# A fused attention and expert kernel: attention steps ordered one deeper, GpSimd's value loads ahead of its stores, squares in pairs, key copies on ScalarE

## What is computed

```python
def _attn_ref(q, k, v):                      # (4, 8, 576, 64) each
    B, H, S, D = q.shape
    window, dilation, scale = 32, 4, 1.0 / np.sqrt(D)
    scores = scale * np.matmul(q, k.transpose(0, 1, 3, 2))
    pos = np.arange(S)
    rel = pos[:, None] - pos[None, :]
    mask_plain = (rel >= 0) & (rel < window)
    mask_dil = (rel >= 0) & (rel < window * dilation) & (rel % dilation == 0)
    masks = np.stack([mask_plain if h < H // 2 else mask_dil for h in range(H)], axis=0)
    scores = np.where(masks[None, :, :, :], scores, -1000000000.0)
    attn = np.exp(scores - np.max(scores, axis=-1, keepdims=True))
    attn = attn / (np.sum(attn, axis=-1, keepdims=True) + 1e-09)
    return np.matmul(attn, v)

x = attention, as rows (2304, 512)
x = moe(x)      # xn = x / norm of the row; expert = argmax(xn @ en.T / tau);
                # gate * relu(x @ w1[e]) @ w2[e]
out = (h * cos(h)) @ w_out, with h = x @ w_in
```

## Time and profile before

| What | Value |
|---|---|
| median of 3 runs | 846.49 us (846.24 to 847.7) |
| the profiled execution | 847.17 us, its span 845.6 us |
| TensorE busy | 820.6 us, 97% of the span |
| VectorE busy | 597.4 us |
| ScalarE busy | 499.5 us |
| GpSimd busy | 95.9 us |
| chain that ended last, TensorE | 88% |
| VectorE's copy of a key block (337) | 460 ns |
| last times V of the attention | about 133.5 us |

### The profile page before, as it was taken

How to read it: one execution, slowest core, us unless ns; L and a number is a source line. 1 busy time by engine, 2 the same in 40 slices (tenths; PEclk the granted TensorE clock), 3 DMA queues, 4 the chain that set the end, 5 groups by cost and what they waited for, 6 DMA issues and landing times.

```text
span 845.6 us, 15742 instructions
## 1 busy us (share of the span) xinstructions
PE 820.6 (97%) x5046; PEld 754.0 (89%) x5046; DVE 597.4 (71%) x1123; ACT 499.5 (59%) x1012; POOL 95.9 (11%) x161
## 2 busy tenths in 40 slices
PE   7999999889999999999999999999999999999995
PEld 6888888789999999999989999989999998999993
DVE  6888887875655555555577777798777788777763
ACT  4677877544544554444566666676666677666652
POOL 3433442340100000000000000011000003000003
PEclk9999999999999999999999999999999999999998
DMA  6687865154544443443422121223121214121001
GB/s 149 146 184 180 196 150 185 41 168 143 187 159 128 150 142 108 150 148 101 157 94 65 61 75 51 75 88 113 51 75 51 76 50 150 51 76 50 26 1 74
DMA packets 109795, 91.44 MB, mean 108 GB/s; under 512 B 60185, under 2 KB 91289, under 8 KB 109729
## 3 DMA queue, kind: packets, MB, share of 16 engines
q1 hardware_dynamic: 103776, 75.01, 30.1%
q0 software_dynamic: 5952, 15.60, 5.9%
HBM read 81.15 MB, written 9.44 MB: 107 GB/s over the span
## 4 chain that ended last, share of the span: by engine, by line
PE 88%; DVE 6%; ACT 2%; issue 2%; POOL 0%; POOLq 0%; ACTq 0%; DVEq 0%
PE bank L783 25%; PE bank L781 25%; PE bank L782 25%; PE bank L620 4%; PE bank L643 3%; PE bank L603 2%; PE bank L629 2%; DVE row_max L1308 1%; DVE shifted L1311 1%; PE bank L616 1%; ACT probs L975 1%; PE bank L823 1%; PE bank L724 1%; DVE xTl L1397 0%; PE bank L699 0%
## 5 line engine op out<-in xcount | busy, mean ns | idle before, releaser
L781 PE MATMUL bank<-yh,up_l 128*128 128x384 f32 x384 | 129.5, 337 | 1.1 <-DVE work L1643 1.1
L783 PE MATMUL bank<-yh,up_h 128*128 128x384 f32 x384 | 129.5, 337 | 0.0
L782 PE MATMUL bank<-yl,up_h 128*128 128x384 f32 x384 | 129.0, 336 | 0.0
L783 PE MATMUL bank<-dn_h,hid 128*128 128x512 f32 x288 | 113.9, 396 | 0.0
L782 PE MATMUL bank<-dn_l,hid 128*128 128x512 f32 x288 | 113.7, 395 | 0.0
L781 PE MATMUL bank<-dn_h,hid 128*128 128x512 f32 x288 | 112.4, 390 | 0.7 <-DVE hid L1636 0.7
L1120 ACT ACTIVATE hid<-bank 128x352 fp32r<-128x352 f32 x64 | 29.7, 465 | 107.7 <-PE bank L783 105.4
L1176 ACT ACTIVATE work<-bank 128x384 f32<-128x384 f32 x96 | 47.2, 491 | 77.4 <-PE bank L783 76.4
L1382 DVE TENSOR_TENSOR dn_l<-dn_raw,dn_h 128x512 fp32r<-128x512 f32 (+1 forms) x79 | 71.8, 908 | 26.7 <-ACT dn_h L1032 24.4
L1188 ACT ACTIVATE work<-work 128x384 f32<-128x384 f32 x96 | 50.5, 526 | 65.1 <-DVE work L1631 63.1
L781 PE MATMUL bank<-xh,up_l 128*128 128x352 f32 x256 | 83.8, 327 | 1.8 <-DVE XS L1517 1.0
(11 more groups left out here) (216 smaller groups left out, 1795.3 us busy)
## 6 DMA issues: line engine op xcount, KB each, us to landing
up_raw<-in_moe_w_dram SPq DMA_DIRECT2D x32, 512.0 KB, 3.6
dn_raw<-in_moe_w_dram SPq DMA_DIRECT2D x32, 512.0 KB, 3.5
up_raw<-in_moe_w_in_dram SPq DMA_DIRECT2D x24, 512.0 KB, 3.5
dn_raw<-in_moe_w_out_dram SPq DMA_DIRECT2D x24, 512.0 KB, 3.6
qn<-in_q_dram SPq DMA_DIRECT2D x32, 144.0 KB, 3.2
kn<-in_k_dram SPq DMA_DIRECT2D x32, 144.0 KB, 3.5
x_rows<-xtok POOLq DMA_DIRECT2D x8, 288.0 KB, 3.4
xtok<-x_rows SPq DMA_DIRECT2D x4, 576.0 KB, 4.6
```

What stands on the lines that cost most here:

```text
L781: mm(o, w[1], x[0], start=first, stop=False, skip_group_check=True)
L782: mm(o, w[0], x[1], start=False, stop=False, skip_group_check=True)
L783: return mm(o, w[0], x[0], start=False, stop=last, skip_group_check=True)
```

## The change

On TensorE the turn of probs goes from one step back to two, times V from two steps back to three, with the same shift on ScalarE (probsT two steps back, the denominators three back, both now ahead of the exponentials) and on VectorE (normalise three back). GpSimd issues the load of the second head's values before it waits for the pair's normalised rows and stores them. The squares stand two at a time in the steps 8, 9 and 11. ScalarE copies all four blocks of the turned keys, and the semaphore `k_head` is gone. The turn of the experts' rows (`experts`) moves from step 4 to step 5.

```diff
-    SQUARE_STEPS = (6, 7, 8, 9, 10, 11)
+    SQUARE_STEPS = (8, 8, 9, 9, 11, 11)
...
+                    if p < PAIRS // 2:
+                        load_second_head(b, p + PAIRS // 2)
                     pool.wait_ge(norm_done, b * STEPS + 3 * p + 7)
...
                         pool.dma_start(xb.rearrange("(t p) c -> p t c", p=QT),
                                        xtok[:, bass.ds(b * NT, NT), 2 * p * D:2 * (p + 1) * D]).then_inc(plain_stored, 16)
-                        load_second_head(b, p + PAIRS // 2)
...
-                    pe.wait_ge(k_head, b * PAIRS + p + 1)
...
                     scores(b, s)
-                    if s == 4:
+                    if s == 5:
                         with pe.If(b < 1):
                             experts()
-                    if s == 5:
+                    if s == 6:
                         pe.wait_ge(embT_ready, 2)
                     if s % 3 == 1:
                         next_pair(b, s, 0)
-                    for lag, stage in ((1, transpose_probs), (2, times_v)):
+                    for lag, stage in ((2, transpose_probs), (3, times_v)):
...
-                half_out(lambda o, x: A(o, x, ACT.Copy), p, 1, first, (0,), k_head)
+                half_out(lambda o, x: A(o, x, ACT.Copy), p, 1, first)
...
                     if s >= 2:
-                        denominators(b, s - 2)
+                        probsT_out(b, s - 2)
...
+                    if s >= 3:
+                        denominators(b, s - 3)
...
                     exps(b, s)
-                    if s >= 1:
-                        probsT_out(b, s - 1)
...
                     if s in SQUARE_STEPS:
-                        before_this(act, b, lambda: squares(b, SQUARE_STEPS.index(s)))
+                        def two_squares():
+                            first = SQUARE_STEPS.index(s)
+                            squares(b, first)
+                            squares(b, first + 1)
+                        before_this(act, b, two_squares)
...
-            def k_out(b, p, first=False):
-
-                dve.wait_ge(s_done, b * STEPS + 3 * p + 3)
-                dve.wait_ge(tr_done, b * 4 * PAIRS + 4 * p + 12)
-                half_out(cp, p, 1, first, (1,))
-
...
-                    if s >= 2:
-                        normalise(b, s - 2)
+                    if s >= 3:
+                        normalise(b, s - 3)
```

More of the change, by code:

```diff
@@ L202, in fused_kernel @@
         tr_out = [sem_from(f"tr_out{i}", 1) for i in range(2)]
-        k_head = sem("k_head")
         init_v = sem("init_v")
@@ L634, in times_v @@
                 pe.wait_ge(norm_done, b * STEPS + (s + 3))
+                whole = 1 if s >= 0 else 0
                 s %= STEPS
@@ L637, in times_v @@
                 if u == 0:
-                    pe.wait_ge(v_in[p % 2], b * (PLAIN_IN + DIL_IN) + (PLAIN_IN if p < 2 else PLAIN_IN + DIL_IN))
+                    pe.wait_ge(v_in[p % 2], (b + whole) * (PLAIN_IN + DIL_IN) if p >= PAIRS // 2 else b * (PLAIN_IN + DIL_IN) + PLAIN_IN)
                     if p >= PAIRS // 2:
-                        pe.wait_ge(head1_v_in[p % 2], (b + 1) * DIL_IN)
+                        pe.wait_ge(head1_v_in[p % 2], (b + whole) * DIL_IN)
                 for i in range(4):
@@ L683, in _ @@
                         next_pair(b, s, 1)
+            transpose_probs(B, -2)
+            times_v(B, -3)
             transpose_probs(B, -1)
@@ L1007, in _ @@
                     if s >= 2:
-                        denominators(b, s - 2)
+                        probsT_out(b, s - 2)
                     else:
-                        before_this(act, b, lambda: denominators(b, s - 2))
+                        before_this(act, b, lambda: probsT_out(b, s - 2))
+                    if s >= 3:
+                        denominators(b, s - 3)
+                    else:
+                        before_this(act, b, lambda: denominators(b, s - 3))
                     exps(b, s)
-                    if s >= 1:
-                        probsT_out(b, s - 1)
-                    else:
-                        before_this(act, b, lambda: probsT_out(b, -1))
                     if s % 3 == 1:
@@ L1018, in _ @@
                     if s in SQUARE_STEPS:
-                        before_this(act, b, lambda: squares(b, SQUARE_STEPS.index(s)))
+                        def two_squares():
[3 more added lines that the diff above has]
+                        before_this(act, b, two_squares)
+            probsT_out(B, -2)
+            denominators(B, -3)
             probsT_out(B, -1)
@@ L1324, in normalise @@
                     rows = osb[p % 2][:, 2 * u:2 * u + 2, :]
-                    if u == 0:
+                    if s == PAIRS // 2 * 3:
                         def slot_stored():
-                            dve.wait_ge(stored[p % 2], b * STORES)
+                            for i in range(2):
+                                dve.wait_ge(stored[i], b * STORES)
                             dve.sem_inc(carrier, 1)
@@ L1337, in over_e @@
                 return x.unsqueeze(2).broadcast_to([QT, RT, E])
-            k_out(0, 0, first=True)
             with dve.Fori(0, B) as b:
@@ L1342, in _ @@
                     shift(b, s)
-                    if s >= 2:
-                        normalise(b, s - 2)
-                    else:
[L1346 to L1352, removed]
+                    if s >= 3:
+                        normalise(b, s - 3)
+                    else:
+                        before_this(dve, b, lambda: normalise(b, s - 3))
                     if s == 1:
@@ L1355, in _ @@
                             emb_rows()
-                    if s == 4:
+                    if s == 5:
                         with dve.If(b < 1):
                             experts_out()
+            normalise(B, -3)
             normalise(B, -2)
```

## The result

The changed kernel is slower by 0.4%, little but clear of the noise: a median of 850.46 us (849.52 to 851.5, 6 runs) against 846.37 (845.83 to 847.99, 6 runs) of the kernel before, ratio 1.004 with a 95% interval of 1.0026 to 1.0055. The forecast was 843.0, the range 841.0 to 845.8. The profiled execution took 849.64, its span is 848.1 us.

The account below looks back on a forecast made before the run. TensorE bounds the kernel, so time is gained where it waits in the attention stage. 4.5 + 0.1 + 0.04 - 0.9 - 0.2 = 3.5 us gained, giving 843.0 from a median of 846.49; range 841.0 to 845.8.

Parts of the forecast that it names:

- the sum: Whole kernel: 4.5 + 0.1 start + 0.04 put off and drain - 0.9 squares - 0.2 guards = 3.5 us gained.
- The turn of probs two steps back: Attention loop: TensorE no longer waits for the exponentials, 40 steps shrink from 100.7 to 96.2 us, gain 4.5.
- Squares in pairs, in the middle: Around step 10 of batches 1 and 2: TensorE waits 0.3 at the key turn, 0.2 at next scores, loss 0.9.
- The walk: Following the engines' queues step by step from e(8)=0: squares' stalls come to 0.46 in each of two batches.
- The drain: After the last scores: 5.1 us to the end of times V, 0.95 longer, about cancelled by 0.99 put off.
- Key copies on ScalarE: Each pair's key turn: all four copies on ScalarE end 0.3 us before they are wanted, so cost nothing.
- e+3.8: Last key copy's end, 3.8 us after e, when a step's scores end on TensorE; wanted at e+4.07.
- the moment of 16.39: First batch: scores(3) start at 16.39 us after the copy of the keys, claimed to stay unchanged.
- The start: From scores(3) to the end of scores(7), first batch: 27.6 instead of 28.6, of which 0.99 only put off, 0.1 gained.
- Values ahead of stores, transfers: Second head's value loads on GpSimd: 7.5 us needed against 8.6 available, so all hidden.
- The rival that transfers set the pace: Attention stage: second heads land 1.5 us later, 8 stops of 0.3 to 0.4, 2.8 back, 845.8; chance 0.18.
- The one in which key copies come last: Each pair's first scores: last key copy 0.8 late, 15 stops of 0.5, 7.5 lost, 849 us; chance 0.08.

Follow-up runs that it names:

- e7_best: Changed kernel with fourth key block on VectorE, squares two in step 8, one each in 9 and 10, last batch's last two behind the attention: 840.45 us, ratio 0.9930.
- e3_vkey: Changed kernel with the fourth key block copied by VectorE again, squares still in pairs: 845.75 us, ratio 1.0006 to the kernel before.
- e5_fill5: Changed kernel with 5 unread identity matmuls between the last turn of probs and the last two times V: 848.92 us, ratio 1.0035 to the kernel before.
- e12_drain: Changed kernel with the last batch's two squares of step 11 moved behind the attention: 845.12 us, ratio 0.9993 to the kernel before.
- e9_before_keys: Kernel before with only all four key blocks copied by ScalarE: 848.61 us, ratio 1.0029.
- e10_before_values: Kernel before with only the second head's values loaded ahead of the store: 845.57 us, ratio 0.9991.
- e4_deeper: Kernel before with only the deeper order, turn of probs two back and times V three back: 851.54 us, ratio 1.0068.
- e6_before_pairs: Kernel before with only the squares in pairs, in steps 8, 9 and 11: 848.93 us, ratio 1.0039.

## Why the prediction was wrong

In the middle the sum had 3.4 gained (4.5 - 0.9 - 0.2), and 1.1 was measured. In the drain it had 0.95 lost, and 3.10 was measured, with another 1.42 in the stage behind it, which the sum put at nothing. Term by term:

**The turn of probs two steps back: right.** The gain of 4.5 in the middle was worked out as 40 steps at 2.07 and 13 pairs of turns at 1.00, 95.8 to 96.2. e7_best, where little else stands in the way, has 96.76, and single steps of 2.05 to 2.08 are in every deeper kernel.

**Squares in pairs, in the middle: right mechanism, term too small.** The walk gave 0.46 for each of two batches, 0.9 in all. Measured: 1.02 at the key turn of each, 2.0 in all; the step after it is 0.2 longer than in batch 0, which has no squares (2.45 against 2.27), and with VectorE's key copy (e3_vkey) it is not longer at all (2.09). One step that failed is the price of a pair: two times 0.62, from 62.63 to 63.25 in the earlier trace rows, where the square that followed another was not in the trace. It is 0.86 with the wait for its neighbour's count, 0.24 more for each pair, and two pairs add up before step 10: 0.5 of the 0.7 by which each stop at the key turn is longer than walked.

**The drain: the step that turned the sign.** The prediction put start and drain together at nought, with 5.1 us from the last scores to the end of times V, against 4.15 before. Measured on the same ends are 7.25 (128.09 to the load at 135.34). Three things are missing in "exponentials end at e+2.1, then two squares ... to e+3.2". VectorE's maximum came 0.8 late behind normalise(7), since its denominator stood behind the squares of step 9, which the walk for batches 1 and 2 had followed on ScalarE but never carried over to VectorE in the last. The pair is 1.5 and not 1.1. And the stops brought the clock down, 2.4 us by e5_fill5, of which 1.04 lie in the drain and 1.36 behind it. The text has no rival in which the granted clock changes, though the stop of 0.80 in the drain of before could have prompted the question what a longer one does. e12_drain shows that this place alone is worth 3.6 us by the stages, as much as the whole loss (3.4 by the stages).

**Key copies on ScalarE: wrong.** "Cover 0.3, so nothing on the path" failed for every pair. The walk had the end of the last copy right: e+3.8, and it stands at e+3.76 before step 6 of batch 1 (54.38). What it had wrong is the moment at which the keys are wanted: e+4.07 is the start of the mask's matmul as the chain has it (65.50 in the earlier trace rows), but it is the weight load that waits, and this stands 0.23 earlier (65.27 in the earlier trace rows). So the keys are wanted at about e+3.8, and the cover is nought. The load then follows the copy by 0.07 at steps 6 and 9, which take 2.11, and by 0.23 at steps 3 and 0, which take 2.35 and 2.27, against 2.09 in e3_vkey. That run puts the whole at 1.4 to 1.6 in the middle, e9_before_keys at 2.97 in the order before. The prediction also said that the moment of 16.39 stays; it came at 16.95, as the first scores of all now stood behind four copies, not three (9.14 against 8.59). The prediction's estimate from the Trainium skill, "ScalarE: Activation LUTs", section "What ACT_TABLE_LOAD costs", would have made the copies 0.3 shorter. The trace shows two key copies in 0.82 us still, so the row was the right one to go by.

**The start: less gained than said.** scores(7) were to be done 1.0 earlier; their mask load stands at 27.20 against 27.34. The stretch from the mask load of scores(3) to it did shrink, from 10.96 to 10.25, and by 1.1 between e10_before_values and the repeat of the changed kernel. The fourth copy of the first keys took 0.56 of it back. Since this stage moves by up to 1.3 us in executions of the same code (27.34 and 28.61), no sharper sum can be made of it.

**Values ahead of stores, transfers: right.** No times V waits for a value after, and e4_deeper shows what would come without. e10_before_values shows that they bring nothing by themselves. The rival that transfers set the pace fell. The one in which key copies come last, given 0.08, was the nearest in kind, since the key copies did come last and squares added to it; but it had 0.5 for each pair where 0.02 to 0.4 were measured, and the larger losses lay at the step with the turns and in the drain.

## What to carry to other kernels

Where a pipeline drains, an engine's side work can stand on the path even if it cost little in the steps before; put it behind the last result, or into the following stage. Price a stop of TensorE twice, once for its length and once for the slower clock that may follow it. In a walk of the queues, take the moment at which something is wanted from the weight load, not from the matmul. A deeper order needs everything that it makes later to be checked by name: here the values, the rows stored and loaded back, and the denominators; each of the edits around it answered one of these, and one was answered in too coarse pieces.

## What was not expected of the hardware

Stops of 0.81 and 1.31 us in a row, with 0.55 us of work between them, were followed by nearly 7 us at 1.2 GHz, in the repeat as well; stops of 0.85 and 0.96 with some 1.3 us of work between them (e6_before_pairs) by 3.4 us; a stop of 0.82 alone (e12_drain) by none. In the first steps, where TensorE also stands still before the first scores, the pace differs between executions. The weight loads of scores(0) and scores(1), and the clock from 9 to 11 us (third number from the end), in e3_vkey:

```profile
8.43 0.81 PEld L621 LDWEIGHTS bank<-kT,qT 128*96 128x96 f32 x4
...
9.51 0.81 PEld L621 LDWEIGHTS bank<-kT,qT 128*96 128x96 f32 x4
...
9.00:11.00 2.00, 2.00 (x14) 1.41 (x13) 1.26 (x2) 0.00 (x0) 1.45 (x10) 1.00 0.61 127
```

and in e10_before_values:

```profile
9.05 1.55 PEld L621 LDWEIGHTS bank<-kT,qT 128*96 128x96 f32 x4
...
11.17 1.56 PEld L621 LDWEIGHTS bank<-kT,qT 128*96 128x96 f32 x4 [0.22 <-issue]
...
9.00:11.00 2.00, 1.99 (x5) 1.37 (x6) 0.00 (x0) 0.48 (x2) 1.43 (x10) 1.00 0.76 140
```

Both read 1.00, yet the second works at half the pace of the first, the pace that the kernel before has at 0.50 (1.56 at 10.52). So the clock column cannot be trusted in these first microseconds, and the duration of like loads can. e3_vkey's is the only one of the fourteen traces in which both these groups of loads take 0.81. The mask load of scores(7) stands between 24.70 and 28.64 us in the fourteen, not only by their code: e10_before_values, whose start is that of the kernel before, has 28.61 against 27.34. This is at least part of the spread of whole runs.

Left open: whether whole runs of e3_vkey are faster than the changed kernel by more than the 1.4 to 1.6 of its stages and the half microsecond or so of the first keys, since the ratios give 2.9 to 3.3 and each is known only to 1.0 to 1.3 us; why e7_best gains 2 us more than its stages show; and why the time from the first expert matmul to the end moves by up to 4.6 us between executions (666.9 to 671.5 us in these traces).
